# Rounded three-term scores from two slots, ScalarE's mask by a steep leaky rectifier, and probabilities scaled on GpSimd

## The reference, cut to what matters

```python
scores = scale * np.matmul(q, k.transpose(0, 1, 3, 2))      # 4 batches, 8 heads, 576 x 576, head size 64
kth = np.partition(scores, -top_k, axis=-1)[..., -top_k:-top_k + 1]      # top_k = 32
scores = np.where(scores >= kth, scores, -1000000000.0)
scores = scores - np.max(scores, axis=-1, keepdims=True)
attn = np.exp(scores)
attn = attn / (np.sum(attn, axis=-1, keepdims=True) + 1e-09)
x = np.matmul(attn, v)                                      # -> 2304 tokens x 512
h = x @ w_in;  g = np.maximum(0.01 * h, h);  x = g @ w_out  # 512 -> 2048 -> 512
h = x @ w_in2; g = np.where(h >= 1, h, np.where(h <= -1, 0.0, (h + 1) ** 2 / 4))
out = g @ w_out2
```

## Time and profile before

| | |
|---|---|
| Median of 3 runs | 1202.42 us (1201.8 to 1202.47) |
| Profiled execution's own time | 1198.35 us |
| Its span | 1196.4 us |
| Mean granted TensorE clock | 0.973 |
| TensorE busy | 1108.2 us, 93% |
| VectorE busy | 924.3 us, 77% |
| ScalarE busy | 701.0 us, 59% |
| GpSimd busy | 608.7 us, 51% |
| DMA | 287.12 MB, mean 240 GB/s |

### The profile page before, as it was taken

How to read it: one execution, slowest core, us unless ns; L and a number is a source line. 1 busy time by engine, 2 the same in 40 slices (tenths; PEclk the granted TensorE clock), 3 DMA queues, 4 the chain that set the end, 5 groups by cost and what they waited for, 6 DMA issues and landing times.

```text
span 1196.4 us, 21062 instructions
## 1 busy us (share of the span) xinstructions
PE 1108.2 (93%) x7360; PEld 999.2 (84%) x7360; DVE 924.3 (77%) x2088; ACT 701.0 (59%) x1579; POOL 608.7 (51%) x582
## 2 busy tenths in 40 slices
PE   3547998899999999999999989999899999999998
PEld 2335887778989988889987978998789999999998
DVE  7999999989799998998989999969989006300234
ACT  5676878756577765666666756566775424312232
POOL 5676778835366643655536744346644323222222
PEclk9758999989999999999999999999999999999999
DMA  6789997766667787767666756455356677787764
GB/s 228 280 300 342 348 346 285 270 229 206 220 223 233 255 285 257 275 230 258 236 233 211 249 182 222 159 198 175 121 194 217 201 256 250 252 283 251 250 239 150
DMA packets 86792, 287.12 MB, mean 240 GB/s; under 512 B 9632, under 2 KB 13472, under 8 KB 86688
## 3 DMA queue, kind: packets, MB, share of 16 engines
q1 hardware_dynamic: 79200, 270.04, 65.5%
q10 hardware_dynamic: 7488, 15.73, 3.9%
HBM read 247.46 MB, written 38.27 MB: 239 GB/s over the span
## 4 chain that ended last, share of the span: by engine, by line
PE 71%; DVE 19%; POOL 3%; issue 3%; ACT 3%; DMA 1%; POOLq 0%; SPq 0%; ACTq 0%
PE ps_f L812 19%; PE ps_f L820 19%; PE ps_f L813 18%; DVE top L1067 7%; DVE work L1070 7%; PE ps_av L771 6%; PE ps_s L727 3%; PE ps_t L748 2%; DVE drop L1076 2%; PE ps_t L727 2%; DVE part_r L1094 2%; PE ps_t L754 2%; POOL gate L644 1%; POOL drop L630 1%; POOL part_o L650 1%
## 5 line engine op out<-in xcount | busy, mean ns | idle before, releaser
L1067 DVE MAX8 top<-work 128x8 f32<-128x576 f32 x432 | 309.3, 742 | 0.1
L812 PE MATMUL ps_f<-xy,w_ring 128*128 128x384 f32 (+2 forms) x896 | 288.8, 322 | 4.5 <-ACT xy L994 2.5
L820 PE MATMUL ps_f<-gate,w_ring 128*128 128x384 f32 (+2 forms) x896 | 281.3, 314 | 9.5 <-POOL gate L644 9.4
L812 PE MATMUL ps_f<-gate,w_ring 128*128 128x384 f32 (+2 forms) x896 | 286.0, 319 | 1.0 <-ACT part_o L975 0.6
L630 POOL TENSOR_TENSOR drop<-scores,drop 128x576 f32<-128x576 f32 x144 | 207.9, 1444 | 150.1 <-DVE drop L1076 150.1
L820 PE MATMUL ps_f<-xy,w_ring 128*128 128x384 f32 (+2 forms) x896 | 280.8, 313 | 1.8 <-POOL xy L654 1.6
L813 PE MATMUL ps_f<-xy,w_ring 128*128 128x384 f32 (+2 forms) x896 | 280.1, 313 | 0.0
L813 PE MATMUL ps_f<-gate,w_ring 128*128 128x384 f32 (+2 forms) x896 | 280.0, 312 | 0.0
L1070 DVE MATCH_REPLACE8 work<-top,work 128x576 f32<-128x576 f32 x288 | 212.7, 739 | 0.0
L812 PEld LDWEIGHTS ps_f<-xy,w_ring 128*128 128x128 f32 x896 | 169.7, 189 | 20.5 <-issue 9.3
L644 POOL TENSOR_TENSOR gate<-part_r,gate 128x384 fp32r<-128x384 f32 (+2 forms) x112 | 101.5, 909 | 157.4 <-ACT gate L979 157.2
(11 more groups left out here) (83 smaller groups left out, 1822.0 us busy)
## 6 DMA issues: line engine op xcount, KB each, us to landing
w_ring<-w_split SPq DMA_DIRECT2D x412, 512.0 KB, 4.2
w_split<-w_ring SPq DMA_DIRECT2D x36, 512.0 KB, 6.0
raw<-wd SPq DMA_DIRECT2D x64, 256.0 KB, 4.3
w_split<-xy SPq DMA_DIRECT2D x28, 512.0 KB, 3.7
kq<-kqd ACTq DMA_DIRECT2D x12, 576.0 KB, 5.8
v_sb<-vd ACTq DMA_DIRECT2D x12, 320.0 KB, 3.2
out_t<-y_acc ACTq DMA_DIRECT2D x12, 192.0 KB, 3.6
kq<-kqd SPq DMA_DIRECT2D x3, 576.0 KB, 6.7
```

The costliest lines, as they stand in the source:

```text
L812: pe.matmul(out, w[:, 0, m], high, start=first, stop=False)
L820: mm = pe.matmul(out, w[:, 0, m], low, start=False, stop=end)
L1067: dve.max(top[:, t % T_SLOTS, 8 * r:8 * r + 8], source(t, r)).then_inc(dve_step, 1)
```

## The change

**The mask.** `neg_max`, `find_drop` and GpSimd's `mask` go, with their buffers. `find_bounds` writes two columns per tile on VectorE: minus the scaled 32nd score, and the scaled difference of the 32nd score and the maximum. ScalarE's `keep` applies a leaky rectifier with slope 1e30 below zero to scale x score - scale x 32nd: kept scores pass, others become hugely negative. `exponential` then works in place with the second column as its bias. **The scaling.** From group 4 on (`starts_early` false) `normalise` runs on GpSimd; the first four groups keep ScalarE's. **The scores.** From group 8 on (`FIRST_ROUNDED`) queries and keys are rounded to a high half (`high_kq`, ScalarE) and a low one (`low_kq`, GpSimd, in two parts), and the scores are three float32r terms. Mixed items now use 128 columns of weights like the others. **The loads.** Keys with queries are laid out per group (832 or 960 columns) in two slots, and values in two slots; all these loads are on SyncE's queue, each with a wait for its slot, ahead of the weight stream of their step.

```diff
+KQ_SLOTS = 2
+V_SLOTS = 2
+KQ_AHEAD = 3
+FIRST_ROUNDED = 8
...
+KQ_FREE = [score_step(ITEMS[FIRST_OF_GROUP[gp]]) - KQ_AHEAD + 1 if gp >= FIRST_ROUNDED else
+           score_step(ITEMS[LAST_SCORED[gp]]) + 1 for gp in range(GROUPS)]
+KQ_LOAD_AT = {KQ_FREE[gp - KQ_SLOTS]: gp for gp in range(KQ_SLOTS, GROUPS)}
+KQ_LOWERED_AT = {score_step(ITEMS[FIRST_OF_GROUP[gp]]) - KQ_AHEAD: gp for gp in range(FIRST_ROUNDED, GROUPS)}
+V_LOAD_AT = {values_step(gp - V_SLOTS) + 1: gp for gp in range(V_SLOTS, GROUPS)}
...
@@ SyncE
+            def load_kq(gp):
+                old = gp - KQ_SLOTS
+                if old >= FIRST_ROUNDED:
+                    sp.wait_ge(kq_low_done, 2 * (old - FIRST_ROUNDED + 1))
+                elif old >= 0:
+                    sp.wait_ge(scores_done, 2 * LAST_SCORED[old] + 2)
...
+            def load_v(gp):
+                if gp >= V_SLOTS:
+                    sp.wait_ge(av_done, gp - V_SLOTS + 1)
...
             for s in range(len(PLAN)):
+                if s in KQ_LOAD_AT:
+                    load_kq(KQ_LOAD_AT[s])
+                if s in V_LOAD_AT:
+                    load_v(V_LOAD_AT[s])
...
@@ GpSimd
-                if READY[0] <= s < TILES + MASK_LAG:
-                    mask(s - MASK_LAG)
+                if s + 1 in OUT_AT and not starts_early(OUT_AT[s + 1].gp):
+                    normalise(OUT_AT[s + 1])
+                if s in KQ_LOWERED_AT:
+                    low_kq(KQ_LOWERED_AT[s], 0)
                 for u in second:
                     event(u)
...
                 for u in third:
                     event(u)
+                if s in KQ_LOWERED_AT:
+                    low_kq(KQ_LOWERED_AT[s], 1)
...
@@ TensorE, score(it)
+                elif it.gp >= FIRST_ROUNDED:
+                    pe.wait_ge(kq_low_done, 2 * (it.gp - FIRST_ROUNDED + 1))
...
+                    terms = [(high, high), (low, high), (high, low)]
...
+                    for n, (q, k) in enumerate(terms):
+                        start, stop = n == 0, n == len(terms) - 1
+                        pe.matmul(out[:, 0, 0:PART], q[0:D, rows[0]], k[0:D, even:even + PART], start=start, stop=stop)
+                        mm = pe.matmul(out[:, 1, 0:PART], q[D:P, rows[1]], k[D:P, odd:odd + PART], start=start, stop=stop)
...
@@ ScalarE
+            def keep(t):
...
+                act.wait_ge(bounds_ready, t + 1)
+                need(act, transposed, it.n - P_SLOTS + 1)
+                act.activation(probs[:, it.n % P_SLOTS, a * S:(a + 1) * S], scores[:, it.n % S_SLOTS, a, :], ACT.Prelu,
+                               bias=bounds[:, t % 8, 0:1], scale=SCALE, alpha=STEEP).then_inc(kept, 1)
...
                 elif s < TILES + EXP_LAG:
-                    exponential(s - EXP_LAG)
+                    keep(s - EXP_LAG)
                 for u in first:
                     event(u)
...
+                elif s < TILES + EXP_LAG:
+                    exponential(s - EXP_LAG)
                 if not scores_first(s):
                     for it in SCORED_AT[s]:
                         copy_scores(it)
-                if s + 1 in OUT_AT:
-                    normalise(OUT_AT[s + 1])
...
+                if s + 1 in KQ_LOWERED_AT:
+                    high_kq(KQ_LOWERED_AT[s + 1])
...
@@ VectorE
+            def find_bounds(t):
...
+                dve.tensor_scalar(bounds[:, t % 8, 0:1], last, -SCALE, None, ALU.mult)
+                dve.tensor_scalar(bounds[:, t % 8, 1:2], last, first, SCALE, ALU.subtract,
+                                  ALU.mult).then_inc(bounds_ready, 1)
```

More of the change, by code:

```diff
@@ L399, in scores_first @@
     return s in OUT_AT
+SCALED_EARLY = sum(starts_early(it.gp) for it in ITEMS)
 SCORED_EARLY = sum(score_step(it) < READY[0] - 1 for it in ITEMS)
@@ L624, in low_direct, with normalise @@
                                    ALU.subtract).then_inc(low_split, 1)
[L626 to L630, removed]
+            def normalise(it):
+                pool.wait_ge(inv_ready, it.n + 1)
+                for a in range(it.tiles):
+                    p = probs[:, it.n % P_SLOTS, a * S:(a + 1) * S]
+                    op = pool.tensor_scalar(p, p, row_inv[:, it.n % T_SLOTS, a:a + 1], None, ALU.mult)
+                op.then_inc(probs_ready_late, 1)
             def low_x(gp):
@@ L655, in low_y, with low_kq @@
                                    ALU.subtract).then_inc(y_low_done, 1)
+            def low_kq(gp, part):
+                pool.wait_ge(kq_high_done, gp - FIRST_ROUNDED + 1)
+                first, end = kq_parts(gp)[part]
+                slot = kq_split[:, gp % KQ_SLOTS, :, first:end]
+                pool.tensor_tensor(slot[:, 1, :], kq[:, gp % KQ_SLOTS, first:end], slot[:, 0, :].bitcast(F32),
+                                   ALU.subtract).then_inc(kq_low_done, 1)
             to_join, to_lower = [], []
@@ L721, in score @@
                     need(pe, p_t_copied, ITEMS_OUT[it.n])
-                q, k = kq[:, it.pair, 0:S], kq[:, it.pair, S:2 * S]
-                for j, out in enumerate(score_halves(it)):
[L724 to L738, removed]
@@ new lines, in score @@
+                if it.gp < FIRST_ROUNDED:
+                    exact = kq[:, it.gp % KQ_SLOTS, :]
+                    terms = [(exact, exact)]
+                else:
+                    high, low = kq_split[:, it.gp % KQ_SLOTS, 0, :], kq_split[:, it.gp % KQ_SLOTS, 1, :]
+                    terms = [(high, high), (low, high), (high, low)]
+                first = it.col + Q_COLS - GROUP_WIDTH[it.group]
+                rows = slice(first, first + P), slice(first, first + P)
+                if it.mixed:
+                    rows = rows[0], slice(first + REST - P, first + REST)
@@ L1033, in _ @@
                     copy_values(CHUNKS[0].last_gp)
+                    keep(s - 1 - EXP_LAG)
                 elif s < TILES + EXP_LAG:
-                    exponential(s - EXP_LAG)
+                    keep(s - EXP_LAG)
                 for u in first:
```

129 lines of the change are left out of this document (68 added, 61 removed).

## The result

The changed kernel takes 1194.81 us (median of 7 runs, 1189.74 to 1196.55), the kernel before beside it 1201.74 us (7 runs). The ratio is 0.9943, 95% interval [0.9925, 0.9961]: 6.9 us faster, where 26 were forecast. The profiled execution took 1194.94 us, its span is 1193.1 us.

What follows compares the result with a forecast made beforehand. VectorE was taken to bound the first stage, partly the second, and TensorE the rest. First stage -6, ramp -6, scores -12, third stage otherwise -2 made -26 us: 1172.4 profiled, 1176.5 as median, range 1165 to 1201.

Steps and rivals of the forecast that it cites:

- new mask: Mask and maximum leave VectorE and GpSimd: 0.36 us less per first-stage tile, first stage -6 us including 0.5 for SyncE's waits.
- ramp: 108 to 245 us, with the first chunk's products: -6 us (range 0 to -11) from the mask's halves going.
- rounded scores: 60 score blocks from group 8 on: 1.17 us each down to 1.00 or 0.92, taken as -12 us.
- scaling on GpSimd: 128 tiles after the first chunk, taken at 1.0 us each, between 0.80 and 1.44; GpSimd's sum -23 us.
- so there is no loss by sum: Third stage: GpSimd, busy 16.74 us in its fullest 20, has room for 1.0 + 0.4 us per tile after 1.44.
- R2: GpSimd stands before the reciprocal or is scaling when TensorE needs a low half: 1192 us, chance 0.18.
- TensorE's waits for GpSimd pass 10 us: A sign that would prove the forecast wrong; third-stage waits for GpSimd's low halves were 5.2 us before.
- R1: Slower: rounded passes of the two row halves don't start together or issue no faster; scores +28, 1216 us, chance 0.12.
- R4: Score blocks keep near their old length by a fixed cost per matmul; 2 us gained, 1186 us, chance 0.05.
- TensorE's first product 5 to 7 us earlier: A sign expected if the forecast holds, beside first-stage VectorE tiles 0.36 us closer.
- The sign that I gave last: First stage: the forecast is wrong if VectorE's sums wait for the exponential; slack there was 0.15 us.
- R3: First two stages bring only 4 us, as ScalarE's order or SyncE's waits become the limit: 1184 us, chance 0.12.

Runs made afterwards that it cites:

- e7: The kernel before with the new mask alone (old loads, float32 scores, ScalarE's scaling): 1183.55 us, ratio 0.9852.
- e6: The changed kernel with ScalarE scaling all probabilities and float32 scores in all groups: 1187.75 us, ratio 0.9875.
- e1: The changed kernel with ScalarE scaling all probabilities, GpSimd none: 1179.68 us, ratio 0.981 to the kernel before.
- e4: The changed kernel with float32 scores in all groups, no rounding, GpSimd's scaling kept: 1195.26 us, ratio 0.9934.
- e8: The changed kernel with GpSimd's scaling as a two-input product, the reciprocal repeated along the row: 1189.48 us, ratio 0.9891.
- e15: The changed kernel with the second tile of GpSimd's scaling moved behind the step's second products, the first tile left: 1193.98 us, ratio 0.9933.
- e3: The changed kernel with every later value load one step later on SyncE's queue: 1191.99 us, ratio 0.9906.
- e11: The changed kernel with ScalarE scaling all tiles and value loads as before (four slots, ScalarE's queue): 1181.39 us, ratio 0.9824.
- e2: The changed kernel with VectorE scaling the 128 later tiles after the reciprocal, GpSimd none: 1205.36 us, ratio 1.0023.
- e5: The changed kernel with ScalarE scaling all probabilities and later value loads one step later: 1181.31 us, ratio 0.9823.

## Why the prediction was wrong

It said 1176.5 us and faster (0.81); it is 1194.8, inside the range of 1165 to 1201 and 18 us over the forecast: 7 us gained, not 26. The parts, each from the kernels that differ by it:

| part | forecast | measured |
|---|---|---|
| new mask (first stage, ramp, third stage) | -14 with the loads | -18 (e7), the new loads +3 to +4 (e6 against e7, weakly) |
| rounded scores | -12 | -8 with ScalarE's scaling (e1 against e6), 0 with GpSimd's (e4) |
| scaling on GpSimd | 0 in the sum | +15 with rounded scores (after against e1), +7.5 without (e4 against e6) |
| sum, with -8 and +15 | -26 | -7 |

**The step that failed is GpSimd's.** It said: 1.0 us a tile, sum -23 us (up to +33), "so there is no loss by sum", and put the scaling at 0. The scaling costs 15 us (e1), and GpSimd's sum went up by 62. The instruction takes 1.73 us, outside my bounds: I took for granted that a one-input instruction is no longer than a two-input one of that size. Here it is longer (1.73 against 1.44, and 1.15 in e8). The Trainium skill (GPSIMD Engine Reference, "4.1 Engine selection") calls one-input work there "roughly line-rate"; the traces disagree for this form, which takes 3.5 times the 0.5 us that I estimated from it.

The excess length cost 5 us (e8). The other 10 are the case that I had as R2, or near it: the scaling stands before something that TensorE needs. I gave it 0.18 and 1192. My argument against it was that GpSimd had waited 150 us for the mask in the same place and TensorE lost only 5.2 us to it. That compared unlike rows: the 150 us are of the whole span, the 5.2 of the third stage and of one named wait; from 108 us on it was 8.9, and 4.9 more of the transposes stood under "issue". The scaling also waits for another thing, the reciprocal (86 us), and then holds GpSimd for 3.5 us of two tiles where the mask held it 1.4. That this difference decides was argued and is not shown: cutting the 3.5 us in two gained nothing (e15). I also looked for the loss in the wrong row. Low halves cost TensorE 5.3 us from 108 to 925 us, less than the 8.9 of before; what came late was the join, and by way of ScalarE's gate copy and the score copies behind it, the transposes. "TensorE's waits for GpSimd pass 10 us" never came true by name: the loss is under "issue". And I priced idle time alone. Some 6 of the 15 us are, by the estimate at e1, the lower clock after the long waits, a term that the sum didn't have.

**Right.** The score block: 0.99 to 1.00 us, pairs 0.13 us apart, 0.18 x 60 = 10.8 us off the blocks. The Trainium skill (TensorEngine Tiling (Array Packing), "Instruction Overhead") has some 60 cycles a matmul, from which I had estimated 0.145 to 0.17 us a pair; 0.13 disagrees with that for such pairs. R1 and R4 are out. The half-group subtractions were said at 1.12 and 1.25 us and took 1.09 and 1.23. The last stage didn't change: the lead is 3.2 us at 925 us and at the end.

**Half right.** "TensorE's first product 5 to 7 us earlier" holds for the values (49.3 to 42.4 us), not for the networks, whose first product came 4.5 us earlier (97.57 to 93.09) and which were 1.1 us ahead by 107 us. In the first stage, then, the lead of 7 us shrinks to 1.1. By the traces of e3 and e11, 2 to 3 us of it went to SyncE's waits for the values' products (16.7 us in three), for which I had charged 0.5. That much is shown in the traces up to 697 us; in the median, e3 has it and e11 has not. The sign that I gave last came true: VectorE's sums wait for the exponential, 3.5 us. The mask without those loads led by 5.2 us at 119, near my -6. The ramp gave 3.7 more, where I had 6, and what follows 6.6, where I had 2 (8.9 at 257 us, 15.5 at the end); with e2 this says that VectorE's work counts in the third stage more than I allowed. R3, with 4 us from the first two stages, fits the kernel without GpSimd's scaling: e1 leads the kernel before by 4.3 us at 257 us, where the forecast had 12, and by 17.5 at the end. ScalarE gained 27 us over the span, where I had 41; its rounding copies took 0.98 us, not 1.1 to 1.3.

Why the rounding gives nothing beside GpSimd's scaling is shown only in part. It puts 55 us of subtractions into the same GpSimd order, as at 503.51 between the scaling and the join. Against e4, the changed kernel loses 6.9 of the 10.8 us at the three places where the scaling's cost falls. Which instruction does it was not tried.

## What to carry to other kernels

Before moving an operation to GpSimd, time that very form there: an instruction of one input isn't bounded by the two-input one. An engine at 63% of a stage can still be the one that is late; ask what stands behind the new instruction in its order, and follow that through the other queues to the engine that bounds. A long wait of that engine can cost more than its length, by the clock after it. And a gain of one part shows only where the next wait lets it: here the shorter scores were worth 8 us or nothing, by where another part ran.

## What the runs showed of the hardware

- GpSimd, 128x576 float32 in SBUF: tensor_scalar by a column 1.73 us, by a constant 1.65 us; tensor_tensor with the column repeated 1.15 us (medians); tensor_tensor of two full inputs 1.44 us (mean). ScalarE scales the same tile in 0.78 us, VectorE in 0.66 us.
- float32r matmuls of 288 columns in two row halves start 0.13 us apart pair after pair, with a weight load for each.
- After the same two gaps of TensorE, 1.7 and 1.4 us (1.1 us nearer each other in e7), its granted clock over the same 10 us was 1.00 (e7), 0.83 (e1), 0.62 (e5) and 0.64 (e11, 688 to 698 us); e5 and e11 came out of it 2.7 and 2.8 us later than e1.
- After an idle gap of 5.2 us the granted clock was 0.51 between 203 and 209 us, and products of 256 columns started 0.21 us apart in place of 0.12.
